# Three more x2 transposes in front of each group's logits, and VectorE's first weight splits held until two gathers are issued

## The chip, the cores and the metric

The kernel runs on one core of a Trainium2 chip. The metric is the device time in microseconds (us) of one execution, lower is better. The profiled execution is a single one of these, with every instruction recorded.

## What is computed

The reference chains three blocks. Their sizes set the work: 1536 tokens of width 512, 8 experts, hidden width 1024.

```python
attn = attention_with_hash_buckets(q, k, v, proj)          # (2, 8, 768, 64)
x    = attn.transpose(0, 2, 1, 3).reshape(1536, 512)
# layer 0: one expert per token, cosine router
logits = normalized(x) @ normalized(expert_emb).T / tau
x2[mask_e] = gate * (relu(x[mask_e] @ w1[e]) @ w2[e])
# layer 1: two experts per token, noisy router
logits = x2 @ w_gate
noisy  = logits + log1p(exp(x2 @ w_noise)) * noise
out[mask_e,k] += gate_k * (relu(x2[mask_e] @ w1[e]) @ w2[e])   # top 2
```

## The kernel before

The program has one instruction stream per engine, written out by hand, and the engines meet in semaphores. The order of work is the order of the code; no scheduler moves anything.

After attention, x lies in SBUF (`x_sb`) and is stored to DRAM as `x_tokens`. VectorE (DVE) then computes the routing of layer 0 in a row of small dependent operations. Their last result is `ids` (L886), the table that says which token rows each expert's tiles hold. It increments `routed`.

**Experts.** `experts(L)` exists once on each engine. For each expert e the tokens are handled as a macro tile of 2 tiles of 128 tokens in layer 0 and 3 in layer 1 (`MTS = (2, 3)`), with a loop over rest tiles where an expert has more tokens. GpSimd (POOL) gathers the rows of each tile from DRAM with one indirect DMA per tile (`gather`, L365, into `xm`). TensorE (PE) transposes a tile (4 matmuls against `ident`, L1203), ScalarE (ACT) copies the result as the high part `xTm_hi` (L569), DVE subtracts to get the low part `xTm_lo` (L897). PE then does the up product (L1249, 96 matmuls), ACT and DVE take the hidden values out as `hT_hi` (L592) and `hT_lo` (L928), and PE does the down product (L1231, 24 matmuls a tile).

**Weights.** Each expert's weights come in 8 chunks of 512 KB (`NCH = 8`): 0 to 3 are w1, 4 to 7 are w2. SP loads a chunk into a ring of 4 buffers `raw` (`RING = 4`, L295). ACT rounds it into `w_hi`, DVE subtracts the rest into `w_lo`, both 128x1024. SP may load chunk G only when both have finished chunk G - 4:

```python
if G >= RING:
    sp.wait_ge(split_hi, G - RING + 1)
    sp.wait_ge(split_lo, G - RING + 1)
sp.dma_start(raw_slot(c), chunk_src(w1, w2, e, c)).then_inc(raw_in[c % RING], 16)
```

Expert 0 of layer 0 is split on its own. ACT makes chunks 0 to 3 at L560, during the routing, and chunks 4 to 7 only behind its two `xTm_hi` copies (L581). DVE makes the low parts of chunks 0 to 3 by `first_low(range(NC1))` (L973) right after the gate table (L994), then the two `xTm_lo` parts, then `first_low` of chunks 4 to 7. From there on each `macro` splits the chunks of the next expert between its evacuations: two chunks, one `hT` part, four times (L581 and L592 on ACT, L918 and L928 on DVE).

**Routing of layer 1.** SP loads the 12 tiles of x2 (256 KB each, L308) into `x_sb`, on a semaphore of its own each (`x2_in[t]`). PE transposes tile t into bank t % 4 of PSUM (L1172, 4 matmuls); from tile 4 on it waits for DVE to be done with tile t - 4 (`rx_ev`). ACT copies it to `x2T_hi` (L631), DVE subtracts into `x2T_lo` (L827). When a group of 4 tiles is complete (`LG = 4`, so three groups), PE computes its logits (`logits`, L1149 x4 and L1152 x4) once `rx_ev` says that the group's last low part is there; ACT copies them out as `logT` (`logits_out`, L624), and PE transposes these back (`logits_back`, L1160 x4). DVE sums all of it at L822 (`r_sum`), the head of the second routing. The buffers `x2T_hi` and `x2T_lo` are double: tile 8 and later, which are group 2, must wait on ACT until the logits of group 0 are done (`lg_ps`).

`keep_clock(n)` (L1140) puts n dummy transposes of `ident` on PE.

Of the kernel before, what the change touches and what calls it, by code (L numbers as in the profile page):

```python
# [15 lines left out]
def attention_moe_kernel(nc, qT, kT, v, proj, expert_emb, tau, m1_w1, m1_w2,  # L16
# [8 lines left out]
    N, DM = noise.shape[0], H * D  # L25
    QC = S // P
    HALF = QC // 2
    NT = N // P
# [6 lines left out]
    MTS = (2, 3)  # L35
# [3 lines left out]
    LG = 4  # L39
# [11 lines left out]
    with ctx:  # L51
# [12 lines left out]
        def sb(name, shape, dt=f32):  # L64
            t = at(name, shape, dt, place[0])
            place[0] += nbytes(shape, dt)
            return t

        def sem(name):
            return ctx.enter_context(nc.semaphore(name))  # L70
# [74 lines left out]
        xm = [sb(f"xm{h}", [P, DM]) for h in range(2)]  # L145
# [51 lines left out]
        rt_act, rt_pe = sem("rt_act"), sem("rt_pe")  # L197
        shift_ready, onehot_ready, slots_ready = sem("shift_ready"), sem("onehot_ready"), sem("slots_ready")
        w_ready, d12_ready = sem("w_ready"), sem("d12_ready")
        routed = sem("routed")  # L200
        raw_in = [sem(f"raw_in{i}") for i in range(RING)]
        split_hi, split_lo = sem("split_hi"), sem("split_lo")
        x2_in = [sem(f"x2_in{i}") for i in range(NT)]
# [124 lines left out]
        def _(pool):  # L328
# [29 lines left out]
            def wait(s, value):  # L358

                pool.wait_ge(s, value)  # L360
                if not isinstance(value, int):
                    pool.sem_inc(pool_pass, 1)

            def gather(dst, idx, rows, s):
                return g.indirect_dma_start(out=dst, out_offset=None, in_=rows,  # L365
                                            in_offset=bass.IndirectOffsetOnAxis(ap=idx, axis=0),
                                            bounds_check=N - 1, oob_is_err=False).then_inc(s, 16)

            def scatter(rows, idx, src, s):
                return g.indirect_dma_start(out=rows, out_offset=bass.IndirectOffsetOnAxis(ap=idx, axis=0),  # L370
# [3 lines left out]
            def experts(L, x_rows, y_rows):  # L374
                s, MT = LS[L], MTS[L]

                def column(e, h):
                    return (idx_m[e % 4] if e else ids)[:, h:h + 1]

                def macro_x(e, r0):  # L380
                    if e:
                        wait(s["xm_ps"], MT * e)
                        for h in range(MT if e > 4 else 0):
                            wait(s[f"ym_out{h}"], 16 * (e - 3))
                        g.tensor_copy(idx_m[e % 4][:, 0:MT], ids[:, bass.ds(r0 + MT * e, MT)]).then_inc(s["idx_m"], 1)
                        wait(s["idx_m"], e)
                    for h in range(MT):
                        gather(xm[h][:], column(e, h), x_rows, s[f"xm_in{h}"])

                def rest_x(k, r, col):  # L390
                    wait(s["xr_ps"], r + 1)
# [58 lines left out]
        def _(act):  # L450
# [176 lines left out]
            for t in range(NT):  # L627
                act.wait_ge(rx_ps, t + 1)
                if t >= 2 * LG:
                    act.wait_ge(lg_ps, t // LG - 1)  # L630
                a.activation(x2T_hi[t // LG % 2][:, :, t % LG * P:(t % LG + 1) * P],  # L631
                             ps[:, t % X2_BANKS, :].rearrange("p (k n) -> p k n", n=P), ACT.Copy).then_inc(rx_hi, 1)
                if t > LG and t % LG == 1:
                    logits_out(t // LG - 1)
            logits_out(NT // LG - 1)
            act.wait_ge(act_table, 2)
# [10 lines left out]
        def _(dve):  # L647
# [322 lines left out]
            def first_low(chunks):  # L970
                for c in chunks:
                    dve.wait_ge(split_hi, c + 1)
                    v_.tensor_tensor(w_lo[0][:, c, :], raw[:, c % RING, :], w_hi[0][:, c, :].bitcast(f32),  # L973
                                     ALU.subtract).then_inc(split_lo, 1)
# [17 lines left out]
            link(v_.reciprocal(gates[:, 0, :], r_s[:]))  # L992
            wide = lambda gate: gate.unsqueeze(2).to_broadcast([P, NT, NX])
            v_.tensor_tensor(gate_tab[:], r_oh[0][:], wide(gates[:, 0, :]), ALU.mult).then_inc(g_ready, 1)  # L994
            first_low(range(NC1))

            experts(0)
# [31 lines left out]
        def _(pe):  # L1029
# [108 lines left out]
            def keep_clock(n):  # L1138
                for _ in range(n):
                    te.transpose(ps[:, 0, 0:P], ident[:], ident[:])  # L1140

            def routing(L):
# [13 lines left out]
                def logits_back(gr):  # L1156

                    pe.wait_ge(lg_ev, gr + 1)
                    for t in range(LG * gr, LG * (gr + 1)):
                        last = te.transpose(ps[:, LOGIT, t * 4 * NX:(t + 1) * 4 * NX], logT[:, t * P:(t + 1) * P],  # L1160
                                            ident[0:4 * NX, 0:4 * NX])
                    last.then_inc(logit_ps, 1)

                if L:
                    keep_clock(44)
                    pe.wait_ge(gate_split, 2)
                    for t in range(NT):
                        pe.wait_ge(x2_in[t], 16)
                        if t >= X2_BANKS:
                            pe.wait_ge(rx_ev, t - X2_BANKS + 1)  # L1170
                        for kk in range(KD):
                            last = te.transpose(ps[:, t % X2_BANKS, kk * P:(kk + 1) * P], x_sb[:, t, kk * P:(kk + 1) * P], ident[:])  # L1172
                        last.then_inc(rx_ps, 1)
                        if t and t % LG == 0:
                            logits(t // LG - 1)
                        if t > LG and t % LG == 2:
                            logits_back(t // LG - 1)
                    logits(NT // LG - 1)
                    logits_back(NT // LG - 1)

                pe.wait_ge(onehot_ready, L + 1)
# [155 lines left out]
```

## Time and profile before

| | us |
|---|---|
| median of 3 runs | 912.56 |
| lowest and highest | 909.87, 912.6 |
| profiled execution, its own time | 911.48 |
| span in its trace | 909.7 |

| engine | busy share of the span |
|---|---|
| TensorE | 90% |
| VectorE | 57% |
| ScalarE | 47% |
| GpSimd | 27% |

The mean granted clock of TensorE in the profiled execution was 0.956 of full speed. The profile names an instruction by its engine and its line in the kernel, the tile that it writes and the one that it reads. "Idle before, releaser" is the time in which the engine stood still ahead of the instruction and the instruction of another engine, or the transfer, that let it go on. The chain of waits is the path through the whole run that ended last. Places in the run are given in us from the span's start.

### The profile page before, as it was taken

To read this page: it belongs to the slowest core of one execution; us is meant where nothing else is said; L and a number is where in the kernel's file an instruction comes from. 1 tells how busy PE (TensorE), PEld (TensorE's weight loads), DVE (VectorE), ACT (ScalarE), POOL (GpSimd) and SP (SyncE) were. 2 spreads that over 40 slices of the span, in tenths; PEclk is the share of its full clock that TensorE was granted. 3 is DMA by queue.
4 is the path that set the end of the run, shared out by engine and by line. 5 is a ranking of instruction groups with operands and counts; after the bars stand their busy time and mean duration, and the time that the engine had idled before them with its cause. 6 is when DMAs were issued, how large, how long until landed. Compare 5 with 4: busy or idle time off the path is not lost.

```text
span 909.7 us, 12779 instructions
## 1 busy us (share of the span) xinstructions
PE 819.3 (90%) x4652; PEld 660.1 (73%) x4652; DVE 520.7 (57%) x884; ACT 423.4 (47%) x689; POOL 248.5 (27%) x247
## 2 busy tenths in 40 slices
PE   4899999999993589999999734999999999999996
PEld 2566566666661579999999623979798997889795
DVE  4788778877865666666666256626253653446221
ACT  5667677787775255555444131415152442425110
POOL 2000000000000313434433001645353664437231
PEclk9899999999997599999999985999999999999999
DMA  5414322130001476766665501725344754355110
GB/s 180 173 70 146 111 73 91 49 119 21 25 1 70 156 266 234 232 231 231 226 228 188 182 1 37 255 74 174 125 133 160 252 175 154 111 186 175 42 43 35
DMA packets 50041, 123.64 MB, mean 136 GB/s; under 512 B 10337, under 2 KB 12385, under 8 KB 49712
## 3 DMA queue, kind: packets, MB, share of 16 engines
q1 hardware_dynamic: 35488, 87.21, 29.0%
q0 software_dynamic: 12032, 29.02, 9.7%
q10 hardware_dynamic: 2448, 6.46, 1.9%
q8 instruction: 44, 0.72, 0.3%
q14 instruction: 29, 0.24, 0.1%
HBM read 109.34 MB, written 17.92 MB: 140 GB/s over the span
## 4 chain that ended last, share of the span: by engine, by line
PE 82%; DVE 8%; DMA 3%; ACT 3%; issue 2%; POOL 1%; ACTq 0%; POOLq 0%; SPq 0%; DVEq 0%
PE ps L1231 27%; PE ps L1249 24%; PE ps L1053 8%; PE ps L1076 7%; PE ps L1062 6%; PE ps L1275 3%; PE ps L1203 2%; PE ps L1043 2%; PE ps L1089 2%; DMA raw<-in_moe_w 1%; DVE row_low L721 1%; DMA xm<-x_tokens,ids 1%; DVE oh_lo L880 1%; ACT probs L473 1%; DVE w_lo L973 1%
## 5 line engine op out<-in xcount | busy, mean ns | idle before, releaser
L581 ACT ACTIVATE w_hi<-raw 128x1024 fp32r<-128x1024 f32 x124 | 129.1, 1055 | 94.4 <-PE ps L1231 75.5
L918 DVE TENSOR_TENSOR w_lo<-raw,w_hi 128x1024 fp32r<-128x1024 f32 x120 | 145.4, 1225 | 39.6 <-ACT w_hi L581 34.0
L1249 PE MATMUL ps<-xTm_hi,w_hi 128*128 128x256 f32 (+1 forms) x512 | 159.9, 312 | 2.9 <-ACT xTm_hi L569 2.9
L1249 PE MATMUL ps<-xTm_lo,w_hi 128*128 128x256 f32 (+1 forms) x512 | 159.6, 312 | 0.0
L1249 PE MATMUL ps<-xTm_hi,w_lo 128*128 128x256 f32 (+1 forms) x512 | 159.6, 312 | 0.0
L1231 PE MATMUL ps<-w_hi,hT_hi 128*128 128x512 f32 x320 | 128.9, 403 | 2.7 <-DVE hT_lo L928 2.7
L1231 PE MATMUL ps<-w_hi,hT_lo 128*128 128x512 f32 x320 | 125.7, 393 | 0.0
L1231 PE MATMUL ps<-w_lo,hT_hi 128*128 128x512 f32 x320 | 125.3, 392 | 0.0
L721 DVE TENSOR_REDUCE row_low<-ps 128x1 f32<-128x768 f32 x96 | 91.7, 956 | 46.6 <-PE ps L1053 45.8
L1053 PEld LDWEIGHTS ps<-K,Q 128*128 128x128 f32 (+1 forms) x384 | 68.2, 198 | 64.1 <-issue 35.9
L473 ACT ACTIVATE probs<-ps,exp_in 128x768 f32<-128x768 f32 x96 | 95.1, 991 | 22.0 <-DVE exp_in L725 22.0
L1053 PE MATMUL ps<-K,Q 128*128 128x512 f32 (+3 forms) x384 | 97.2, 377 | 8.4 <-DMA Q<-row_bits_Q 4.0
L1249 PEld LDWEIGHTS ps<-xTm_hi,w_hi 128*128 128x128 f32 x512 | 98.9, 193 | 4.1 <-ACT xTm_hi L569 3.5
L365 POOL DMA_INDIRECT xm<-x_tokens,ids x5 | 7.0, 1409 | 346.3 <-DVE ids L886 345.4
L1249 PEld LDWEIGHTS ps<-xTm_lo,w_hi 128*128 128x128 f32 x512 | 98.7, 193 | 0.5
L1249 PEld LDWEIGHTS ps<-xTm_hi,w_lo 128*128 128x128 f32 x512 | 98.7, 193 | 0.0
L480 ACT ACTIVATE probsT<-ps 128x512 f32<-128x512 f32 x96 | 57.0, 594 | 55.5 <-PE ps L1062 54.4
L1062 PE MATMUL ps<-ident,probs 128*128 128x128 f32 x576 | 81.9, 279 | 0.8 <-ACT probsT L480 0.6
L569 ACT ACTIVATE xTm_hi<-ps 128x512 fp32r<-128x512 f32 x40 | 23.9, 598 | 123.4 <-PE ps L1203 123.4
L592 ACT ACTIVATE hT_hi<-ps 128x384 fp32r<-128x384 f32 (+1 forms) x96 | 50.3, 524 | 65.4 <-PE ps L1249 58.7
L1076 PE MATMUL ps<-probsT,v 128*64 128x384 f32 x384 | 80.0, 514 | 0.0
L1062 PEld LDWEIGHTS ps<-ident,probs 128*128 128x128 f32 x576 | 65.8, 142 | 15.4 <-issue 14.3
(227 smaller groups left out, 1137.2 us busy)
## 6 DMA issues: line engine op xcount, KB each, us to landing
raw<-in_moe_w SPq DMA_DIRECT2D x128, 512.0 KB
rows_K<-in_k SPq DMA_DIRECT2D x8, 768.0 KB, 4.4
rows_Q<-in_q SPq DMA_DIRECT2D x8, 768.0 KB, 5.8
v<-in_v SPq DMA_DIRECT2D x8, 384.0 KB, 3.5
out<-xr ACTq DMA_DIRECT2D x1, 3072.0 KB, 14.6
x_tokens<-x_sb ACTq DMA_DIRECT2D x2, 1536.0 KB, 5.1
x_sb<-x_tokens SPq DMA_DIRECT2D x12, 256.0 KB, 5.1
K<-row_bits_K SPq DMA_DIRECT2D x24, 24.0 KB
```

What stands on the lines that cost most here:

```text
L473: a.activation(probs[s % 2][:], ps[:, sc:sc + 2, :].rearrange("p a n -> p (a n)")[:, 0:S], ACT.Exp, bias=exp_in[:, s % 2, 1:2], scale=exp_ ...
L480: a.activation(probsT[hf][:, 0:NA, head, cq * P:(cq + 1) * P], ps[:, PTA, 0:NA * P].rearrange("p (c n) -> p c n", n=P), ACT.Copy).then_inc ...
L581: a.activation(w_hi[E % 2][:, c, :], raw[:, c % RING, :], ACT.Copy).then_inc(split_hi, 1)
L592: a.activation(hT_hi[:, FC * i:FC * (i + 1), 0:TW], ps[:, n % UP_BANKS, 0:FC * TW].rearrange("p (k n) -> p k n", n=TW), ACT.Relu).then_inc ...
L721: v_.tensor_reduce(lows[:, 1:2], ps[:, sc:sc + 2, :].rearrange("p a n -> p (a n)")[:, 0:S], AX.X, ALU.min)\
L918: v_.tensor_tensor(w_lo[E % 2][:, c, :], raw[:, c % RING, :], w_hi[E % 2][:, c, :].bitcast(f32), ALU.subtract).then_inc(split_lo, 1)
L1053: last = te.matmul(ps[:, bank, 0:hi - lo], opd[a_][b][0:rows, head, cq * P:(cq + 1) * P], opd[b_][b][0:rows, head, lo:hi], start=(i == 0), ...
L1062: last = te.transpose(ps[:, bank, i * P:(i + 1) * P], probs[s % 2][:, kc * P:(kc + 1) * P], ident[:])
L1076: last = te.matmul(ps[head * D:(head + 1) * D, OB, 0:HALF * P], vv[b][:, head, kc, :], probsT[hf][:, kc, head, :], start=(kc == 0), stop=( ...
L1231: last = te.matmul(ps[:, bank, :], x_[:, fc, cols], w_[par][:, c, w], start=(fc == 0 and i == 0), stop=(fc == KF - 1 and i == 2))
L1249: last = te.matmul(ps[:, n % UP_BANKS, j * TW:(j + 1) * TW], w_[par][:, kk, f], x_[:, kk, 0:TW], start=(kk == 0 and m == 0), stop=(kk == K ...
L1275: last = te.matmul(ps[:, H0 + hf, :], x_[:, kk, :], w_[par][:, kk, w], start=(kk == 0 and i == 0), stop=(kk == KD - 1 and i == 2))
```

## The change

Two places are edited. First, in the routing of layer 1, `logits(0)` and `logits(1)` are issued behind the transposes of tiles 6 and 10 instead of 4 and 8, and the results of the first two groups are transposed back later; the last group's calls stay at the end, behind them. ACT's `logits_out` of group 0 comes behind its copy of tile 7 instead of 5, of group 1 behind 11 instead of 9. Second, in layer 0, the two indirect DMAs of expert 0 increment a new semaphore `x_issued` by one each through `engine_sem`, and DVE waits for 2 of them ahead of `first_low(range(NC1))`.

```diff
@@ semaphores @@
-        routed = sem("routed")
+        routed, x_issued = sem("routed"), sem("x_issued")
@@ GpSimd @@
-            def gather(dst, idx, rows, s):
+            def gather(dst, idx, rows, s, issued=None):
                 return g.indirect_dma_start(out=dst, out_offset=None, in_=rows,
                                             in_offset=bass.IndirectOffsetOnAxis(ap=idx, axis=0),
-                                            bounds_check=N - 1, oob_is_err=False).then_inc(s, 16)
+                                            bounds_check=N - 1, oob_is_err=False, engine_sem=issued).then_inc(s, 16)
...
-                        gather(xm[h][:], column(e, h), x_rows, s[f"xm_in{h}"])
+                        gather(xm[h][:], column(e, h), x_rows, s[f"xm_in{h}"], x_issued if e == L == 0 else None)
@@ ScalarE @@
-                if t > LG and t % LG == 1:
+                if t > LG and t % LG == LG - 1:
                     logits_out(t // LG - 1)
@@ VectorE @@
             v_.tensor_tensor(gate_tab[:], r_oh[0][:], wide(gates[:, 0, :]), ALU.mult).then_inc(g_ready, 1)
+            dve.wait_ge(x_issued, MTS[0])
             first_low(range(NC1))
@@ TensorE @@
                         last.then_inc(rx_ps, 1)
-                        if t and t % LG == 0:
+                        if t > LG and t % LG == 2:
                             logits(t // LG - 1)
-                        if t > LG and t % LG == 2:
-                            logits_back(t // LG - 1)
+                        if t > 2 * LG and t % LG == 1:
+                            logits_back(t // LG - 2)
                     logits(NT // LG - 1)
+                    logits_back(NT // LG - 2)
                     logits_back(NT // LG - 1)
```

The first order listing is TensorE's, in the routing of layer 1, from the transposes of x2 tile 4 (`x2_in4`) on. Before:

```order
L1172 MATMUL ps<-ident,x_sb 128x128 [waits rx_ev,x2_in4]
L1172 MATMUL ps<-ident,x_sb 128x128 x3
L1149 MATMUL ps<-x2T_hi_154,gate_hl 32x512 [waits rx_ev]
L1149 MATMUL ps<-x2T_hi_154,gate_hl 32x512 x3
L1152 MATMUL ps<-x2T_lo_156,gate_hl 16x512 x4
L1172 MATMUL ps<-ident,x_sb 128x128 [waits rx_ev,x2_in5]
L1172 MATMUL ps<-ident,x_sb 128x128 x3
L1172 MATMUL ps<-ident,x_sb 128x128 [waits rx_ev,x2_in6]
L1172 MATMUL ps<-ident,x_sb 128x128 x3
L1160 MATMUL ps<-ident,logT 128x32 [waits lg_ev]
L1160 MATMUL ps<-ident,logT 128x32 x3
```

The same stretch of TensorE in the changed kernel, whose lines are one higher there:

```order
L1173 MATMUL ps<-ident,x_sb 128x128 [waits rx_ev,x2_in4]
L1173 MATMUL ps<-ident,x_sb 128x128 x3
L1173 MATMUL ps<-ident,x_sb 128x128 [waits rx_ev,x2_in5]
L1173 MATMUL ps<-ident,x_sb 128x128 x3
L1173 MATMUL ps<-ident,x_sb 128x128 [waits rx_ev,x2_in6]
L1173 MATMUL ps<-ident,x_sb 128x128 x3
L1150 MATMUL ps<-x2T_hi_154,gate_hl 32x512 [waits rx_ev]
L1150 MATMUL ps<-x2T_hi_154,gate_hl 32x512 x3
L1153 MATMUL ps<-x2T_lo_156,gate_hl 16x512 x4
L1173 MATMUL ps<-ident,x_sb 128x128 [waits rx_ev,x2_in7]
L1173 MATMUL ps<-ident,x_sb 128x128 x3
```

Tiles 5 and 6 now stand ahead of the first group's logits, and the first `logits_back` has moved out of this stretch, behind the transposes of tile 9.

On VectorE, behind the gate table of layer 0, the order before was:

```order
L994 TENSOR_TENSOR gate_tab<-r_oh_171,gates 128x96 [waits dve_step]
L973 TENSOR_TENSOR w_lo_112<-raw,w_hi_110 128x1024 [waits split_hi] x4
L897 TENSOR_TENSOR xTm_lo<-ps,xTm_hi 128x4x128 [waits xm_hi_l0] x2
L973 TENSOR_TENSOR w_lo_112<-raw,w_hi_110 128x1024 [waits split_hi] x4
L918 TENSOR_TENSOR w_lo_113<-raw,w_hi_111 128x1024 [waits split_hi] x2
```

It is now:

```order
L994 TENSOR_TENSOR gate_tab<-r_oh_171,gates 128x96 [waits dve_step]
L973 TENSOR_TENSOR w_lo_112<-raw,w_hi_110 128x1024 [waits split_hi,x_issued]
L973 TENSOR_TENSOR w_lo_112<-raw,w_hi_110 128x1024 [waits split_hi] x3
L897 TENSOR_TENSOR xTm_lo<-ps,xTm_hi 128x4x128 [waits xm_hi_l0] x2
L973 TENSOR_TENSOR w_lo_112<-raw,w_hi_110 128x1024 [waits split_hi] x4
```

Nothing is reordered on VectorE; the first of the eight splits has one wait more.

## Rows read from the trace of the kernel before

**Rows 1.** The chain that ended last, shares of the span by engine.

```profile
PE 82%; DVE 8%; DMA 3%; ACT 3%; issue 2%; POOL 1%; ACTq 0%; POOLq 0%; SPq 0%; DVEq 0%
```

**Rows 2.** Stretches: us, PE, PEld, DVE, ACT, POOL busy, granted clock, DMA share, GB/s.

```profile
340.00:506.00 166.00, 166.00 (x1073) 151.15 (x1072) 101.42 (x110) 78.67 (x96) 65.02 (x61) 1.00 0.66 220
306.00:311.00 5.00, 1.05 (x6) 0.81 (x7) 0.69 (x1) 0.60 (x1) 0.00 (x0) 0.72 0.96 348
516.00:520.00 4.00, 3.12 (x14) 2.59 (x15) 2.06 (x4) 1.79 (x3) 0.00 (x0) 0.57 1.01 361
```

**Rows 3.** Timeline of GpSimd, gathers of both layers: start, us, instruction, idle before.

```profile
301.16 2.22 POOL L365 DMA_INDIRECT xm<-x_tokens,ids  x1 [295.11 <-DVE ids L886]
303.69 1.77 POOL L365 DMA_INDIRECT xm<-x_tokens,ids  x1 [0.31 <-issue]
...
315.74 1.96 POOL L365 DMA_INDIRECT gate_r<-gates,ids  x1 [0.30 <-issue]
...
562.15 1.00 POOL L365 DMA_INDIRECT xm<-x_tokens,ids  x1 [0.30 <-issue]
```

**Rows 4.** Timeline of VectorE, the eight splits of expert 0.

```profile
301.10 4.62 DVE L973 TENSOR_TENSOR w_lo<-raw,w_hi 128x1024 fp32r<-128x1024 f32 x4
...
313.33 4.63 DVE L973 TENSOR_TENSOR w_lo<-raw,w_hi 128x1024 fp32r<-128x1024 f32 x4 [0.25 <-ACT w_hi L581]
```

**Rows 5.** Timeline of TensorE, the head of expert 0 and of layer 1's first.

```profile
310.61 1.11 PE L1203 MATMUL ps<-ident,xm 128*128 128x128 f32 x4 [3.20 <-DMA xm<-x_tokens,ids]
313.18 0.55 PE L1249 MATMUL ps<-xTm_hi,w_hi 128*128 128x256 f32 x1 [1.46 <-ACT xTm_hi L569]
...
565.88 0.66 PE L1203 MATMUL ps<-ident,xm 128*128 128x128 f32 x4 [0.59 <-DMA xm<-x_tokens,ids]
```

**Rows 6.** Timeline of the SP queue: chunk 4 of expert 0, chunk 0 of expert 1.

```profile
302.40 0.37 SPq L295 DMA_DIRECT2D raw<-in_moe_w  x1
...
314.63 0.34 SPq L295 DMA_DIRECT2D raw<-in_moe_w  x1
```

**Rows 7.** Timeline of ScalarE: the first splits behind the gathers and behind new chunks.

```profile
312.25 3.88 ACT L581 ACTIVATE w_hi<-raw 128x1024 fp32r<-128x1024 f32 x4
319.47 1.06 ACT L581 ACTIVATE w_hi<-raw 128x1024 fp32r<-128x1024 f32 x1 [3.33 <-DMA raw<-in_moe_w]
```

**Rows 8.** The chain in order of time, 303 to 344: start, us, what.

```profile
303.69 6.88 DMA xm<-x_tokens,ids
...
318.04 6.11 DMA raw<-in_moe_w
...
334.16 0.61 DVE hT_lo L928
```

**Rows 9.** Timeline of TensorE in the routing of layer 1.

```profile
516.32 2.78 PE L1172 MATMUL ps<-ident,x_sb 128*128 128x128 f32 x12 [1.23 <-DMA x_sb<-x_tokens]
519.66 1.16 PE L1149 MATMUL ps<-x2T_hi,gate_hl 128*32 128x512 f32 x4 [0.56 <-DVE x2T_lo L827]
...
521.59 1.03 PE L1172 MATMUL ps<-ident,x_sb 128*128 128x128 f32 x8
...
525.77 1.11 PE L1149 MATMUL ps<-x2T_hi,gate_hl 128*32 128x512 f32 x4 [0.97 <-DVE x2T_lo L827]
...
531.82 1.11 PE L1149 MATMUL ps<-x2T_hi,gate_hl 128*32 128x512 f32 x4 [1.41 <-DVE x2T_lo L827]
```

**Rows 10.** Timelines there of ScalarE (first row) and VectorE (second).

```profile
522.22 0.60 ACT L631 ACTIVATE x2T_hi<-ps 128x512 fp32r<-128x512 f32 x1 [2.48 <-PE ps L1172]
...
535.00 0.56 DVE L822 TENSOR_REDUCE r_sum<-ps 128x192 f32<-128x384 f32 x1 [3.24 <-PE ps L1160]
```

**Rows 11.** The loads of x2: the SP queue's issues, and issue to landing.

```profile
511.00 5.85 SPq L308 DMA_DIRECT2D x_sb<-x_tokens  x12
...
DMA to landing us min/median/max: 2.7/5.1/5.8
```

**Rows 12.** The low parts of x2 on VectorE, all 12.

```profile
L827 DVE TENSOR_TENSOR x2T_lo<-ps,x2T_hi x12: 680/692/692, 515.1 to 531.1; 128x512 fp32r<-128x512 f32 x12
```

## The prediction

> **What bounds the kernel now.** I read the chain of waits first: TensorE carries 82% of it [rows 1], so time is to be had only where TensorE stands still. A stretch table shows that it does not from 340 to 506, where it is busy for 166.00 of 166.00 us [rows 2]. What starts earlier by some us at 340 therefore ends earlier by as much at 506, and the reverse. The two edits lie in the two gaps around this stretch, and each can be worked out alone.
>
> *Gap A, 300 to 344, head of expert 0.* GpSimd issues the two gathers at 301.16 and 303.69 and takes 2.22 and 1.77 us for them; the same instruction takes 1.00 at the head of layer 1 [rows 3]. What differs is VectorE, which runs four splits of 1.16 us each beside them from 301.10 to 305.72 [rows 4]; in layer 1 it has no split to do there. The first split also frees a ring slot, so SP issues chunk 4 at 302.40 [rows 6], ahead of the second gather. From 306 to 311 the DMA engines are 96% busy at 348 GB/s [rows 2], and the second gather, issued at 303.69, lands 6.88 us later [rows 8]. TensorE waits 3.20 us for it and starts the up product only at 313.18 [rows 5].
> That start isn't what ends the gap. ScalarE makes chunks 4 to 7 behind its `xTm_hi` copies, from 312.25 [rows 7]; VectorE follows at 313.33 [rows 4]; only then may SP load expert 1 (314.63, [rows 6]). The chain goes through these loads, one of them 6.11 us long, to the `hT_lo` part at 334.16 that the down product needs [rows 8]. So the gap's length is set by when chunks 4 to 7 are split.
>
> *Gap B, 511 to 535, routing of layer 1.* Three times TensorE stands before a group's logits waiting for the low part of the group's last tile: 0.56, 0.97 and 1.41 us [rows 9]. Only then does it do the logits and the next transposes, so ScalarE and VectorE stand still meanwhile: ScalarE 2.48 us ahead of tile 5 [rows 10]. Each engine waits in turn. The end is `r_sum` at 535.00 [rows 10].
>
> **The change, part A.** No instruction is added but one wait. The gathers now run beside small operations only, so I take the layer 1 price, 1.00 each with 0.31 between [rows 3]: they end at 302.2 and 303.5 instead of 303.4 and 305.5. The splits start at about 303.6 instead of 301.1: **2.5 us later**, the price. Queued behind them are the two `xTm_lo` parts and chunks 4 to 7 on VectorE, and SP, which waits for the first split with chunk 4 (now about 304.9).
> Landing: the last gather of layer 1's head ended its issue at 563.15 [rows 3] and its tile was transposed from 565.88 on [rows 5], 2.7 us later. That puts the second gather at 306.2 instead of 310.56. Its transposes take up to 1.11 [rows 5], its copy 0.60, so ScalarE is free for chunk 4 at about 307.9 instead of 312.25. VectorE ends the first splits at 308.2 and the `xTm_lo` parts at 309.6, where TensorE starts the up product: 3.6 us earlier.
> But chunk 4 is late next. The nearest load, chunk 0 of expert 1, took 4.84 us from issue (314.63) to ScalarE's start (319.47) [rows 6, 7]. By that chunk 4 lands at 309.7 and shifts by -2.55, not -4.4. Chunk 7, issued about 3.4 us behind chunk 4, lands at 313.1, or some 0.6 later because expert 1's gathers (two of 256 KB at 348 GB/s are 1.5 us of transfer) now fall among these loads. ScalarE and VectorE need 1.06 and 1.16 us on it: 316.0 instead of 317.96, so -2. The chain runs through the load that this frees (318.04), and with fewer gathers beside it that load should take less than 6.11. Taking -2 for the chunk and 0.4 for the lighter queue, **A = -2.4 us**. Bounds: -4 if chunk 4 lands as soon as ScalarE is free, -0.5 if the gathers stay slow (below).
> The earlier start of the up product is worth nothing by itself: TensorE then waits longer for `hT_lo`.
>
> **Part B.** The same 96 matmuls, in another order; 12 tiles stay 12 tiles. Worked out from tile 4 on, whose transposes end at 519.1 as before [rows 9]:
> - Tiles 5 and 6 need low parts 1 and 2, long done, and their loads. Their issues are 0.49 us apart from 511.00 and land 5.1 us later in the median, 5.8 at most [rows 11]; tile 6 lands at about 519. TensorE runs at half clock here (0.57 from 516 to 520, [rows 2]), and a tile costs 0.9, at full clock 0.52 (8 matmuls in 1.03, [rows 9]). Both end at 520.3.
> - Logits 0 need low part 3 (519.6): no wait. They take 2.0 (519.66 to the next transposes at 521.59), to 522.3. Meanwhile ScalarE and VectorE do tiles 5 and 6; that is the gain.
> - Tiles 7, 8, 9 follow to 523.6; ScalarE copies tile 7 at 522.9, `logT` at 523.4, then 8 and 9. TensorE waits 0.4 for `logT`, transposes back (0.43), does tile 10 and reaches logits 1 at 524.9; low part 7 was done at 524.2. They end at 526.9, tile 11 at 527.3.
> - ScalarE and VectorE add 0.60 and 0.69 [rows 10, 12] with the small gaps before: low part 11 at 528.7. TensorE waits 1.4 for it. This last wait stays, since nothing is left to put in front.
> - Logits 2 end at 530.8, `logT` at 531.4, and the transposes back at 531.9; those of group 1 hide under that copy. `r_sum` starts at 531.9 instead of 535.00: **B = -3.1 us**.
> Bounds: -3.8 if tiles 5 and 6 go at full clock, -1.3 if logits 0 stay at half clock, where 4 matmuls of 512 columns take twice the 1.1 us (+1.8).
>
> **A rule that speaks against the change.** The slow gathers stand beside VectorE's two-input subtractions [rows 3, 4]. The Trainium skill (SBUF — State Buffer, Who interferes with whom) says that `tensor_tensor` takes only the shared pair's read interface and infers that it doesn't stall descriptor generation, which needs the write interface. By it the gathers would be slow for a reason of their own, and the sum would be that of the first rival.
>
> **Sum.** A -2.4, B -3.1: -5.5 us. From the profiled execution's own time, 911.48, that is 906.0. The median of the runs shown is 1.1 us above that execution and the lowest 1.6 below; I keep the sum.
>
> **The rivals.**
> 1. *The gathers are slow by themselves*, for instance since they are the first of the program. For it: those of layer 1 come when the code has long been run. Against it: the indirect DMA of `gate_r` at 315.74, no longer the first, takes 1.96 beside the splits of [rows 4], on a table of 8 values a row [rows 3]. They would end at 305.46 as now, the splits would start there, 4.4 later, chunk 4 would land at 306.75 + 4.84 = 311.6 against 312.25, and A would be -0.6: 907.8.
> 2. *The clock takes part of B.* The half-clock stretch around 516 to 520 [rows 2] ends later, or a new one comes in gap A's longer wait for `hT_lo`. One group of logits at half clock costs 1.8, two such stretches 3.6: 908 to 909.6.
> 3. *Slower: the wait lasts until the gathers have landed*, and they land no sooner than now. VectorE starts at 310.6, chunk 4 is issued at 311.8 and lands at 316.7, or 317.9 with 6.11; against 312.25 A is +4.4 to +5.7, with B +1.3 to +2.6: 912.8 to 914.1. It decides from the point where the splits start behind 309.2 (A above +3.1). Against it: the semaphore is attached to the issuing engine, and without the ring's loads in front nothing holds the gathers up.
> 4. *The reordering does nothing*, since the loads of x2 are the limit. Against it: the last is issued at 516.4 and landed by 522.2 [rows 11], 5 us ahead of its new use at 526.9. B = 0 would give 909.1.
>
> **How the numbers follow.** The forecast gets 0.72 (its own range 903.8 to 908.0), rival 1 0.10, rival 2 0.10, rival 3 0.03, rival 4 0.05. About 0.3% (2.7 us) is what a measurement of this kernel tells from no change. Faster by more than that: the forecast, rival 1 and half of rivals 2 and 4, 0.89; within it their other halves and a part of rival 3, 0.09; slower, rival 3 with a stretch at half clock on top, 0.02. Range 903.3 to 909.3: A and B at their favourable bounds less a little for the spread of the runs, up to rival 4.
>
> **What would show it.** Right: two gathers of about 1.0 us, the first split at 303.6, the up product at about 309.6, chunks 4 to 7 now waiting on ScalarE for their loads, `hT_lo` at about 331.8; in the second gap one wait of some 1.4 us left before logits, and `ids` to `r_sum` shorter by 3. Wrong: gathers still of 2 us, a first split behind 305, TensorE waiting for `x_sb` loads behind tile 4, or a granted clock of 0.5 at the first logits.

## The result and the profile after

| us | before | change |
|---|---|---|
| first comparison, median (lowest to highest) | 911.21 (909.35 to 912.6) | 901.68 (901.49 to 903.07) |
| median of all runs of the study (84 and 21) | 910.4 | 902.4 |
| profiled execution, its own time | 911.48 | 901.77 |
| span in its trace | 909.7 | 899.9 |
| mean granted clock of TensorE | 0.956 | 0.964 |

The first comparison gave a ratio of 0.990 with an interval of 0.9875 to 0.9925; two later ones of the unchanged files gave 0.9921 (0.9897 to 0.9945) and 0.9917 (0.9885 to 0.9949). The change is worth about -8 us. Both 902.4 and the 901.68 of the first comparison lie below the forecast range of 903.3 to 909.3.

The chain that ended last, shares of the span by engine, of the change:

```profile
PE 82%; DVE 8%; DMA 3%; issue 2%; ACT 2%; POOL 1%; ACTq 0%; SPq 0%; POOLq 0%; DVEq 0%
```

The shares are those of before [rows 1] but for ScalarE's, 2% for 3%; they don't show where the gain lies. That is read from the two gaps. The head of expert 0, GpSimd's timeline:

```profile
299.77 1.19 POOL L365 DMA_INDIRECT xm<-x_tokens,ids  x1 [293.72 <-DVE ids L886]
301.27 1.00 POOL L365 DMA_INDIRECT xm<-x_tokens,ids  x1 [0.31 <-issue]
...
309.44 1.13 POOL L365 DMA_INDIRECT gate_r<-gates,ids  x1 [0.30 <-issue]
```

VectorE's, from the same point (first split, fourth `hT_lo` part), and behind it `r_sum` of the second gap:

```profile
302.31 4.63 DVE L973 TENSOR_TENSOR w_lo<-raw,w_hi 128x1024 fp32r<-128x1024 f32 x4 [2.52 <-DMA xm<-x_tokens,ids]
...
328.98 0.68 DVE L928 SCALAR_TENSOR_TENSOR hT_lo<-ps,hT_hi 128x512 fp32r<-128x512 f32 x1
...
525.50 0.56 DVE L822 TENSOR_REDUCE r_sum<-ps 128x192 f32<-128x384 f32 x1 [3.23 <-PE ps L1161]
```

The SP queue's issue of chunk 4:

```profile
303.62 0.37 SPq L295 DMA_DIRECT2D raw<-in_moe_w  x1
```

ScalarE, which now waits for the chunks themselves:

```profile
307.40 1.06 ACT L581 ACTIVATE w_hi<-raw 128x1024 fp32r<-128x1024 f32 x1 [1.48 <-DMA raw<-in_moe_w]
...
311.78 1.06 ACT L581 ACTIVATE w_hi<-raw 128x1024 fp32r<-128x1024 f32 x1 [0.29 <-DMA raw<-in_moe_w]
```

TensorE, the transposes of the second gathered tile and the first up matmul:

```profile
304.62 0.66 PE L1205 MATMUL ps<-ident,xm 128*128 128x128 f32 x4 [0.62 <-DMA xm<-x_tokens,ids]
...
308.24 0.36 PE L1251 MATMUL ps<-xTm_hi,w_hi 128*128 128x256 f32 x1 [2.96 <-DVE xTm_lo L897]
```

The gathers cost 1.19 and 1.00 us instead of 2.22 and 1.77 [rows 3], and TensorE waits 0.62 instead of 3.20 for the second tile [rows 5]. The indirect DMA of `gate_r` cost 1.13 instead of 1.96, although VectorE has splits beside it here too (from 308.49 to 311.04).

Times from the span's start can't be compared between traces as they stand: `ids` falls at 300.07 in the trace of before and at 298.68 here, and over all traces at 297.0 to 300.1 where nothing ahead of it is edited. So from here on places in the first gap are counted from `ids`, and those in the second from "the last y", the `ym` (L912) by which VectorE takes out the last down product of layer 0 (499.98 in the trace of the change). Between the two, from expert 1's up product to the last y, every trace of either kernel has 162.85 to 162.94 us.

TensorE in the second gap, of the change:

```profile
509.59 4.53 PE L1173 MATMUL ps<-ident,x_sb 128*128 128x128 f32 x20 [0.51 <-DMA x_sb<-x_tokens]
513.77 1.34 PE L1150 MATMUL ps<-x2T_hi,gate_hl 128*32 128x512 f32 x4
...
515.87 1.47 PE L1173 MATMUL ps<-ident,x_sb 128*128 128x128 f32 x12
517.62 0.43 PE L1161 MATMUL ps<-ident,logT 32*128 32x32 f32 x4 [0.28 <-ACT logT L624]
517.98 0.66 PE L1173 MATMUL ps<-ident,x_sb 128*128 128x128 f32 x4
518.39 1.16 PE L1150 MATMUL ps<-x2T_hi,gate_hl 128*32 128x512 f32 x4
...
522.33 1.11 PE L1150 MATMUL ps<-x2T_hi,gate_hl 128*32 128x512 f32 x4 [1.41 <-DVE x2T_lo L827]
```

Of the three waits for low parts, 0.56, 0.97 and 1.41 us [rows 9], the last is left, as forecast.

### The profile page after: what moved, and what is told of

Its sections match the earlier page's. It is cut to its first block, busy times and chain, and to the rows that moved or that the text cites. A ratio compares the mean times of both kernels' runs of the same rounds, so it can differ in the third digit from the quotient of the medians.

```text
span 899.9 us, 12780 instructions
## 1 busy us (share of the span) xinstructions
PE 814.1 (90%) x4652; PEld 655.8 (73%) x4652; DVE 521.1 (58%) x884; ACT 424.2 (47%) x689; POOL 243.9 (27%) x247
## 4 chain that ended last, share of the span: by engine, by line
PE 82%; DVE 8%; DMA 3%; issue 2%; ACT 2%; POOL 1%; ACTq 0%; SPq 0%; POOLq 0%; DVEq 0%
PE ps L1233 27%; PE ps L1251 24%; PE ps L1054 8%; PE ps L1077 7%; PE ps L1063 6%; PE ps L1277 3%; PE ps L1044 2%; PE ps L1205 2%; DMA raw<-in_moe_w 2%; PE ps L1090 2%; DVE row_low L721 1%; PE ps L1173 1%; DVE oh_lo L880 1%; DVE w_lo L973 1%; DMA xm<-x_tokens,ids 1%
## 5 line engine op out<-in xcount | busy, mean ns | idle before, releaser
L365 POOL DMA_INDIRECT xm<-x_tokens,ids x5 | 5.2, 1049 | 341.7 <-DVE ids L886 340.8
```

## The experiments

Each was built on one of the two kernels and profiled once. Logits 0 are the first four matmuls of L1149 (L1150 in the change). The times by part, in us:

| kernel | `ids` to 4th `hT_lo` | `hT_lo` to expert 1's up | last y to logits 0 | logits 0 to `r_sum` | `r_sum` to `ids` of layer 1 |
|---|---|---|---|---|---|
| before | 34.00 | 9.74 | 13.00 | 15.34 | 23.49 |
| e3, before again | 34.35 | 8.14 | 12.76 | 15.72 | 23.49 |
| e8, dummies | 34.33 | 8.13 | 12.36 | 16.73 | 23.48 |
| e10, idle wait | 34.35 | 8.15 | 12.53 | 15.50 | 23.10 |
| e2, order only | 34.58 | 8.14 | 12.53 | 11.59 | 23.48 |
| e1, wait only | 32.22 | 9.73 | 12.29 | 16.57 | 23.09 |
| e5, load held | 32.69 | 9.72 | 12.56 | 16.60 | 23.50 |
| e6, wait for one | 31.02 | 8.14 | 12.90 | 15.33 | 23.09 |
| e7, wait for landing | 33.87 | 9.68 | 12.80 | 18.22 | 23.10 |
| after | 30.30 | 8.13 | 13.79 | 11.73 | 23.09 |
| e4, change again | 30.26 | 9.67 | 13.15 | 11.59 | 23.09 |
| e9, change again | 31.17 | 8.15 | 13.51 | 11.60 | 23.10 |
| e16, change again | 29.93 | 8.14 | 13.77 | 11.58 | 23.11 |
| e12, splits on GpSimd | 30.03 | 9.67 | 12.89 | 11.60 | 23.09 |
| e11, 66 dummies | 32.70 | 9.77 | 12.51 | 11.59 | 23.10 |
| e15, 66 dummies | 30.51 | 8.34 | 13.05 | 11.57 | 23.12 |
| e13, four in front | 31.18 | 8.16 | 14.04 | 8.98 | 23.12 |
| e14, four and 66 | 30.76 | 8.13 | 13.67 | 8.97 | 23.10 |

### The two halves and the repeats: e1 to e4, e9, e16

e1 has the second edit alone: `x_issued`, its two increments and VectorE's wait. e2 has the first alone: the order of `logits`, `logits_back` and `logits_out`. e3 is the kernel before, and e4, e9 and e16 the change, unedited.

> VectorE's wait for the two gathers alone, TensorE's order as before. Counted from ids (L886), so that drift ahead of it doesn't enter. Theory 1 (the two edits are independent and the first is worth more than I gave it): hT_lo's last part of expert 0 comes 30.4 us behind ids instead of 34.1, the routing of layer 1 keeps its 28.3 us, and the time falls by 4 to 6 us. Theory 2 (the first edit is worth the 2.4 us of the prediction and the rest is drift of the run): hT_lo at 31.7 behind ids or the time falls by 2 to 3 us only.

> TensorE's and ScalarE's new order in the routing of layer 1 alone. Theory 1 (as predicted): from the last ym (L912) of layer 0 to r_sum 25.5 us instead of 28.3, the stretch from ids to expert 1's up product unchanged at 43.9, the time falls by 2.5 to 3.5 us. Theory 2 (the order gives only what the clock allows): 26.5 us or more where TensorE is at half clock in front of the first logits, a fall of under 2 us.

> The kernel before, profiled once more, as a measure of what one trace differs from the next. If the 1.39 us by which ids came earlier in the changed kernel's trace is drift of TensorE's clock in the attention part, ids lands anywhere between 298.5 and 300.5 here; if it belongs to the change, it lands at 300.1 again. The gathers take 2.2 and 1.8 us again, and the half-clock stretch at expert 0's down product shows whether it is there every time.

> The changed kernel, profiled once more. Theory 1 (the 1.6 us between hT_lo and expert 1's up product belong to the change, since TensorE's wait falls otherwise): TensorE at full clock from 329 to 337 again, expert 1's up product 8.2 us behind hT_lo. Theory 2 (chance of the clock): a stretch at half clock there, 9.8 us. ids to expert 1's up product 38.6 by the first, up to 40.2 by the second.

> The changed kernel in many runs, since four runs stand against twelve of each half. The halves alone gave -3.9 and -4.3 us. Theory 1 (they add up): -8.2, a median of 902.3 where the kernel before has 910.5. Theory 2 (together they give more, for instance since the clock falls less): under 901.5.

> The changed kernel again. By the sum of the parts seen in the traces (hT_lo 3.0 earlier behind ids, the routing of layer 1 4.1 shorter, the pause at r_w 0.4) it is 7.5 us below the kernel before, a ratio of 0.992; if the first comparison (0.990) was right, 9 us. hT_lo 30.3 to 32.7 behind ids, first logits to r_sum 11.6.

Measured, medians: e1 906.65 against 910.52, ratio 0.996 (0.9941 to 0.9979), so -3.9. e2 906.26, 0.9958 (0.9938 to 0.9978), -4.3. Together -8.2, the change's -8: the two halves add up. Each median is beyond the forecast of its half (-2.4 and -3.1), but the intervals, -5.4 to -1.9 and -5.7 to -2.0, take in both forecasts. Of e1's two theories neither fits whole: the time fell by nearly the 4 us of the first, while `hT_lo` came 32.22 behind `ids`, later than either had it. e2 beat its first theory: from the last y to `r_sum` 24.12 instead of 25.5. e3 took 908.93 and e4 900.55, once each; single runs say little, since those of before in the same comparison go from 907.0 to 914.04. e9 had a median of 902.84 against 909.92, e16 903.16 against 909.43, as the sum of the halves had it.

The repeats show what one trace can't. Before's own logits 0 to `r_sum` varies from 15.33 to 16.73, once 18.22, in traces with nothing changed there. The clock makes most of it. In the four long traces (e1, e5, e7, e8: 16.57 to 18.22) the last four matmuls of L1149 take 1.91 or 1.92 us, in the four short ones (15.33 to 15.72) 1.11 or 1.12. This is e1's trace. First its timeline, then its stretch around that point (PE, PEld, DVE, ACT, POOL busy, granted clock, DMA share, GB/s):

```profile
526.23 1.91 PE L1150 MATMUL ps<-x2T_hi,gate_hl 128*32 128x512 f32 x4 [1.41 <-DVE x2T_lo L827]
```

```profile
526.00:528.00 2.00, 1.77 (x5) 0.72 (x6) 0.18 (x1) 0.00 (x0) 0.00 (x0) 0.50 0.00 0
```

The same four matmuls took 1.11 in [rows 9]. In the new order this part is 11.6 to 11.7 in every trace that has it.

### Why the gathers were slow: e5 and e6

Two things leave the gathers' neighbourhood when VectorE waits: its splits, and SP's load of chunk 4, which the first split frees. e5 keeps the splits where they were in before and holds the load instead; e6 waits for one gather only. Both, and e7 below, keep the old order in the second gap.

```diff
# e5: the kernel before, with x_issued, and in SP's loads
+                if G == RING:
+                    sp.wait_ge(x_issued, MTS[0])
# e6: against the change
-            dve.wait_ge(x_issued, MTS[0])
+            dve.wait_ge(x_issued, 1)
```

> VectorE's splits start at once as before, but SP issues chunk 4 only when both gathers are issued. Computation unchanged. Theory 1 (most of the gain of the first edit is that the gathers stand ahead of the ring's loads): the gathers still take 2.2 and 1.8 us to issue beside the splits, the second tile is transposed at about 8.2 us behind ids (10.5 before, 6.0 changed), chunk 4 is issued at 5.5 behind ids against 4.9, hT_lo comes at 30.8 to 31.3, and the time falls by nearly as much as with VectorE's wait alone. Theory 2 (it is the gathers' faster issue that counts): the second tile stays later than 9.5 behind ids, hT_lo at 33 or later, a fall of 1 us or none.

> VectorE waits for the first gather's issue only. Theory 1 (splits slow whatever gather they run beside): the first gather takes 1.2 us, the second 1.8 again; the splits start 2.3 behind ids instead of 3.6, chunk 4 is issued 1.3 us earlier; the second tile is transposed at about 7.5 to 9 behind ids. hT_lo at 29.5 to 31, since chunk 4's landing sets it. Theory 2 (a gather behind ring loads is what hurts): second tile at 10 behind ids again, and hT_lo at 33 or more.

GpSimd's timeline of e6:

```profile
299.72 1.19 POOL L365 DMA_INDIRECT xm<-x_tokens,ids  x1 [293.67 <-DVE ids L886]
301.22 1.83 POOL L365 DMA_INDIRECT xm<-x_tokens,ids  x1 [0.31 <-issue]
```

The first gather, without splits beside it, is the fast one; the second, beside them, is slow, in one and the same run. In e5 the loads are held and the splits run as before:

```profile
299.76 2.21 POOL L367 DMA_INDIRECT xm<-x_tokens,ids  x1 [293.71 <-DVE ids L888]
302.28 1.78 POOL L367 DMA_INDIRECT xm<-x_tokens,ids  x1 [0.31 <-issue]
```

So the issue of the two gathers is slowed by the splits, not by the loads, and not by their being the first. The inference weighed in the prediction (the Trainium skill, SBUF — State Buffer, Who interferes with whom: `tensor_tensor` leaves the write interface free, hence descriptor generation) doesn't hold for this pair: the indirect DMAs pay 1.03 and 0.77 us beside the splits. The price isn't the same for every one. This gather of before stands wholly beside the splits of 313.33 to 317.96 [rows 4], and it paid 0.24:

```profile
314.20 1.24 POOL L365 DMA_INDIRECT xm<-x_tokens,idx_m  x1 [0.30 <-issue]
```

What sets the price, no run here tells.

The landing is another matter. TensorE's transposes of the second tile, in e5:

```profile
306.38 1.11 PE L1205 MATMUL ps<-ident,xm 128*128 128x128 f32 x4 [1.43 <-DMA xm<-x_tokens,ids]
```

They start 7.71 behind `ids` instead of 10.54 in before and 5.94 in the change. The issues of e5 are as slow as before's, so 2.8 of the 4.6 us by which the second tile comes earlier are had by keeping the ring's loads from going out ahead of it, and 1.8 by the faster issues.

For the time, e6 had a median of 906.48, ratio 0.997 (0.9948 to 0.9992), the same as e1: one waited-for gather is enough, with `hT_lo` at 31.02. e5 had 908.74 against 909.92, 0.9984 (0.9962 to 1.0007), which can't be told from no change, although its `hT_lo` comes at 32.69, 1.6 earlier than before. So its first theory was right on the gathers and the second tile, its second on the time.

### What the delay of the splits costs: e7

Here, on the kernel before, VectorE waits until both gathers have landed:

```diff
+            for h in range(MTS[0]):
+                dve.wait_ge(LS[0][f"xm_in{h}"], 16)
```

> VectorE waits until both gathers have landed, not only until they are issued (the third rival's mechanism, by itself). Theory 1 (hT_lo follows chunk 4's issue one for one): the splits start at about 5.9 behind ids instead of 3.6, chunk 4 goes out 2.3 us later, hT_lo at 32.6 and a gain of 1.5 to 2 us over the kernel before. Theory 2 (as the third rival had it, later than before): hT_lo above 34.3 and a time above the kernel before's.

The first split starts 6.01 behind `ids` instead of 3.63, `hT_lo` comes at 33.87, and the median is 913.26, ratio 1.002 (0.9992 to 1.0047). The 2.4 us took back the whole gain; that they cost more than that isn't clear of the noise. Neither theory fits whole: `hT_lo` is later than the first had it (32.6) and earlier than the second (34.3), and the gain of 1.5 to 2 us isn't there. ScalarE's timeline shows the price, a wait for chunk 4:

```profile
310.51 1.06 ACT L581 ACTIVATE w_hi<-raw 128x1024 fp32r<-128x1024 f32 x1 [3.81 <-DMA raw<-in_moe_w]
```

Its trace also has the longest second gap, 18.22, where no edit was made. By its parts up to `hT_lo` e7 should be near the kernel before; why the median of ten runs lies 3.3 above it is open.

### The clock ahead of expert 1: e8

From `hT_lo` to expert 1's up product the traces show 8.1 or 9.7 us, but for e15's 8.34. Stretches in the down product, of before, of the change and of e4:

```profile
336.00:338.00 2.00, 2.00 (x8) 1.71 (x7) 0.56 (x1) 0.60 (x1) 0.00 (x0) 0.50 0.80 264
```

```profile
330.00:332.00 2.00, 2.00 (x12) 1.64 (x12) 0.47 (x2) 0.60 (x1) 0.00 (x0) 1.00 0.93 313
```

```profile
330.00:332.00 2.00, 2.00 (x8) 1.61 (x8) 0.20 (x1) 0.00 (x0) 0.00 (x0) 0.50 0.95 338
```

The change and e4 are the same file: after the wait for `hT_lo` the granted clock is at its full 2.4 GHz in one and at 1.2 GHz in the other. e8 puts dummies into before's waits there:

```diff
+                            if E == 0 and h == 0 and fc in (4, 6):
+                                for _ in range(4 if fc == 4 else 20):
+                                    te.transpose(ps[:, YR, 0:P], ident[:], ident[:])
```

> The kernel before with 4 and 20 dummy transposes of ident into an idle bank, where TensorE waits for the third and fourth hT_lo of expert 0 (some 0.5 and 2.2 us). From hT_lo to expert 1's up product the traces so far show either 8.14 or 9.7 us, in kernels with and without the change. Theory 1 (it is the clock, which falls in that wait in some executions): the granted clock stays at 1.00 through the down product and the stretch is 8.1. Theory 2 (something else): 9.7 at full clock. No theory gives more than 1.6 us of the whole.

The part took 8.13, at clock 1.00, and e8 took 909.99 in its one run against a median of 912.13. But e3 and e10 reach 8.14 and 8.15 without dummies. So the run agrees with the dummies keeping the clock and doesn't show it. The 1.6 us difference that the first pair of traces has here goes with the clock, which either kernel has at either level, and is no part of the change's worth.

### A pause that moved: e10

In the change, `r_sum` to `ids` of layer 1 is 23.09 instead of 23.49, with no edit there. VectorE, before and then after:

```profile
536.37 0.21 DVE L1002 TENSOR_SCALAR r_w<-r_u 128x96 f32<-128x96 f32 x1 [0.81 <-ACT r_u L639]
```

```profile
526.48 0.21 DVE L1003 TENSOR_SCALAR r_w<-r_u 128x96 f32<-128x96 f32 x1 [0.42 <-ACT r_u L639]
```

e10 adds to before one wait that is met already, ahead of `first_low(range(NC1))`:

```diff
+            dve.wait_ge(routed, 1)
```

> The kernel before, with a wait on VectorE at the place of the new one, on a semaphore that is long there (routed, 1). From r_sum to ids of layer 1 the kernels with a wait at that place took 23.09 us and those without 23.49. Theory 1 (one more instruction moves VectorE's later code, and a pause in front of r_w goes with it): 23.09 here too, the gathers slow as before (2.2 and 1.8 us), hT_lo at 34. Theory 2 (the 0.4 comes from the earlier state of the engines): 23.49.

23.10, with everything else as before; its one run took 908.0. In before, e2, e3, e5 and e8, where VectorE's instructions are as they were, it is 23.48 to 23.50; wherever one wait or two were added, 23.09 to 23.12. e12, below, adds none and has four splits fewer on VectorE, and there it is 23.09 too. So it isn't the waiting: one instruction more or four fewer far ahead takes 0.4 off a pause some 225 us later. That those behind it then lie at other addresses would fit; no run here settles it.

### Moving splits to GpSimd: e12

On the change, GpSimd makes the four low parts ahead of its wait for the stores of `x_tokens`, during the routing, and VectorE's wait and its first four splits go:

```diff
+            for c in range(NC1):
+                wait(split_hi, c + 1)
+                g.tensor_tensor(w_lo[0][:, c, :], raw[:, c % RING, :], w_hi[0][:, c, :].bitcast(f32),
+                                ALU.subtract).then_inc(split_lo, 1)
...
-            dve.wait_ge(x_issued, MTS[0])
-            first_low(range(NC1))
```

ScalarE's splits of chunks 4 to 7 stand ahead of its wait for the gate table.

> The changed kernel, but GpSimd makes the low parts of chunks 0 to 3 during the routing of layer 0, when it has nothing to do, and ScalarE makes chunks 4 to 7 ahead of the gate table. VectorE's first four splits and its wait go. Theory 1 (gap A is the ring of four buffers turning): chunks 4 to 7 are loaded 10 us or more before ids, expert 1's loads start at about 10 behind ids instead of 10.7 to 12, and hT_lo at 26 to 29, until TensorE's own work (13.9 for the up product behind 8.2) becomes the bound; a gain of 2 to 5 us over the changed kernel. Theory 2 (GpSimd's subtractions hold VectorE's routing up, or are so slow that they hold the gathers up): ids later by more than 2 us counted from the last row maximum, or the first gather later than 1.1 behind ids, and no gain.

909.54 against 912.13 is 0.9975 (0.9949 to 1.0001), so most of the gain of the change is gone, as its second theory had it. `hT_lo` came 30.03 behind `ids`, no earlier than in the change, where the first theory had 26 to 29. First GpSimd, then VectorE beside it:

```profile
285.62 9.24 POOL L446 TENSOR_TENSOR w_lo<-raw,w_hi 128x1024 fp32r<-128x1024 f32 x4 [279.56 <-ACT w_hi L564]
```

```profile
285.95 2.05 DVE L668 TENSOR_SCALAR r_s<-r_nrm 128x12 f32<-128x12 f32 x1
288.03 0.23 DVE L669 RECIPROCAL r_s<-r_s 128x12 f32<-128x12 f32 x1
...
290.33 2.26 DVE L671 TENSOR_TENSOR r_s<-r_s,r_nrm 128x12 f32<-128x12 f32 x1
...
294.92 0.17 DVE L985 TENSOR_SCALAR r_nrm<-r_nrm 128x12 f32<-128x12 f32 x1
```

Four operations on 12 elements a partition take 2.00 to 2.26 us beside GpSimd's, 0.17 once it is done, and `ids` comes 7.9 us later (23.51 behind the row of sums `r_ssq`, against 15.62). So it goes both ways: VectorE's splits slow GpSimd's gathers, and GpSimd's splits hold up VectorE. That VectorE shares a pair of ports with GpSimd is what the same section of the Trainium skill describes, and this trace agrees.

### The clock at the second gap: e11 and e15

The new order starts logits 0 later, behind two more tiles. `keep_clock(44)` became `keep_clock(66)`; e11 and e15 are the same file.

> The changed kernel with 66 dummy transposes instead of 44 ahead of the routing of layer 1, which fills 2.3 us more of TensorE's wait for the first tile of x2. Theory 1 (the half-clock stretch that sets in while TensorE waits for x2 is what B varies by): TensorE is at full clock through the first logits, from the last ym to r_sum 24.1 us (the best seen) instead of 24.7 to 25.5, and 0.5 to 1.4 us off the median. Theory 2 (the later wait, for tile 2, drops the clock anyway, or the dummies hold the first transposes up): 24.7 or more, no gain.

> The changed kernel with 66 dummy transposes once more, in more runs. Theory 1: the first logits start 12.5 us behind the last ym instead of 13.2 to 13.8, so 0.5 to 1.3 us below e16, the changed kernel on the same chip. Theory 2 (the one trace at 12.5 was chance, as the kernels before had it too): no difference from e16.

901.54 and 901.33, ratios 0.9877 (0.9822 to 0.9932) and 0.99 (0.9872 to 0.9928); beside e15 on the same chip the change had 903.16. Last y to logits 0 was 12.51 and 13.05 against 13.15 to 13.79 in four traces of the change. By the stretch from 508 to 510 of the change's trace, the clock is down while it waits for x2:

```profile
508.00:510.00 2.00, 1.49 (x7) 1.09 (x7) 0.95 (x2) 1.19 (x2) 0.00 (x0) 0.50 0.98 345
```

The direction fits, but the intervals overlap, and e2 (12.53) and e12 (12.89), with the new order and 44 dummies, start logits 0 as early: a gain of up to 1 or 2 us, not settled.

### Taking the last wait away too: e13 and e14

The change has three tiles in front of the logits of groups 0 and 1, where before had one (so two more, not three as the title has it), and none in front of group 2's. It leaves 1.41 us ahead of the last logits. e13 puts one more tile in front of the logits of groups 0 and 1, and all three `logits_back` behind the last logits; e14 has 66 dummies as well.

```diff
-                        if t > LG and t % LG == 2:
+                        if t > LG and t % LG == LG - 1:
                             logits(t // LG - 1)
-                        if t > 2 * LG and t % LG == 1:
-                            logits_back(t // LG - 2)
                     logits(NT // LG - 1)
+                    logits_back(NT // LG - 3)
```

> The changed kernel with one more tile in front: logits of group 0 behind tile 7, of group 1 behind tile 11, and the results transposed back only behind the last logits. Theory 1 (it is the order): tile 11's low part is made while TensorE does the logits of group 1, so the last wait of 1.41 us ahead of the logits of group 2 goes, and the first transposes back are off the path as well. First logits start 0.5 us later, first logits to r_sum 9.3 us instead of 11.6: 1.5 to 2 us off the changed kernel. Theory 2 (ScalarE, which may copy tiles 8 and later only behind the first logits, becomes the bound): tile 11's low part is still late, and the sum changes by less than 0.5.

> The same with 66 dummy transposes ahead of the tiles of x2 instead of 44. Theory 1 (the clock): from the last ym to the first logits 13.0 us instead of up to 14.3, at full clock, and 0.5 to 1 us less than e13 in the median. Theory 2: no difference.

TensorE in e13:

```profile
515.69 1.18 PE L1150 MATMUL ps<-x2T_hi,gate_hl 128*32 128x512 f32 x4
...
517.65 1.91 PE L1173 MATMUL ps<-ident,x_sb 128*128 128x128 f32 x16
519.32 1.18 PE L1150 MATMUL ps<-x2T_hi,gate_hl 128*32 128x512 f32 x4
...
521.49 1.11 PE L1150 MATMUL ps<-x2T_hi,gate_hl 128*32 128x512 f32 x4
...
523.46 1.18 PE L1161 MATMUL ps<-ident,logT 32*128 32x32 f32 x12
```

No row waits: the logits of group 1 now fill the 1.41 us in which VectorE makes the last low part. Logits 0 to `r_sum` is 8.98 instead of 11.6, while logits 0 starts about 0.5 later than in the change (14.04 against a mean of 13.56 in its four traces). The median is 900.34, 0.9883 (0.9854 to 0.9912), against the change's 903.16 on the same chip. e14 had 898.58, 0.9878 (0.9843 to 0.9913), the lowest median of the study, 4.6 below the change's on the same chip and 3.8 below that of all the change's runs. Its interval and e13's overlap almost wholly, and e13's overlaps a little with the change's own of 0.9885 to 0.9949; what carries the verdict on the fourth tile is the part from logits 0 to `r_sum`, 8.98 and 8.97. Whether the 66 dummies add to it isn't shown.

## Why the prediction was wrong, by its steps

The direction was right, and so was each of the two mechanisms in the main. Two terms of the sum were too small, the loads behind chunk 4 in gap A and the time that gap B had before. Means over traces, against the forecast, in us:

| term | forecast | measured | from |
|---|---|---|---|
| A, gap of expert 0 | -2.4 | -3.3 | 34.3 (5 traces without a wait or held load) to 31.0 (9 with the full wait) |
| B, second gap | -3.1 | -4.0 | 28.9 (8 with the old order) to 24.9 (6 with the new, 44 dummies) |
| `r_w`'s pause | none | -0.4 | 23.5 to 23.1 |
| sum | -5.5 | -7.7 | the medians say -8.0 |

B leans on e7's 18.22: without that trace the old order has 28.6, and B is -3.7.

The rest of the distance from 906.0 to 902.4 is the base: the profiled execution, at 911.48, lay 1.1 above the median of 84 runs. The first comparison's own difference, 9.5, is in turn 1.5 more than all runs together show, and part of that is luck. Between the spans of its two traces, 9.8 apart, A is -3.7, the clock ahead of expert 1 -1.6, B -2.8, `r_w`'s pause -0.4, and `ids` falls 1.4 earlier with no edit ahead of it. So in that pair B came out a little under the forecast, and 3.0 of the 9.8 us are no work of the change.

**Gap A, the front.** Counted from `ids`, the forecast had the first split at 3.5, chunk 4's issue at 4.8 and the up product at 9.5; they came at 3.63, 4.94 and 9.56. The gathers cost 1.19 and 1.00 against 1.00 each. Rival 1 (slow by themselves) is refuted by e6. Rival 3 (the wait lasts until landing) didn't happen, and e7 shows what it would have cost: the gain, with no clear loss.

**Gap A, the loads: the first step that failed.** "By that chunk 4 lands at 309.7." I took its landing from chunk 0 of expert 1, 4.84 us [rows 6, 7]; it took 3.78, from the issue at 303.62 to ScalarE's start at 307.40. That is 8.7 behind `ids` instead of 9.6, and it is 8.6 to 8.7 in all nine traces with the full wait: half the way to the favourable bound, where ScalarE is free (7.8). The load that chunk 7 frees, at 318.04 in before and 17.97 behind `ids`, went out 15.49 behind it, 2.5 earlier instead of 2. And the term of 0.4 for "the lighter queue" was too small. The chain of the change has these loads:

```profile
307.01 4.75 DMA raw<-in_moe_w
...
314.17 5.28 DMA raw<-in_moe_w
...
321.87 4.85 DMA raw<-in_moe_w
```

The last two, 5.28 and 4.85, stand where before had 6.11 [rows 8] and 5.25: 1.2 us where the forecast had 0.4. The two terms, 2.5 and 1.2, are the -3.7 of this pair. The loads vary: e5's chain has one of 6.97, and `hT_lo` with the full wait comes anywhere from 29.9 to 32.7. So how the 0.9 by which the mean -3.3 exceeds the forecast is shared between the two isn't known. The mean lies inside the bounds -4 to -0.5; I took too little of it.

**Gap B: the new order's time was right, the old one's was not.** Logits 0 were to start 0.6 later and did (12.65 to 13.27 in the means of traces that go from 12.29 to 13.79, so the agreement is in part luck). From there to `r_sum` I had 531.9 - 520.3 = 11.6, and six traces have 11.58 to 11.73. Three waits less one, the free start of logits 0 and 1, and the last 1.41 us all came as worked out. (Tiles 7 to 9 at 0.52 each end at 523.9, not 523.6; the wait for `logT` takes that up, and it was 0.28 instead of 0.4.) What failed is the value it was set against: 15.34 of the one trace is with e6's 15.33 the lowest of eight, whose mean is 16.25 (15.97 without e7), since in four of them the clock is down behind the old order's last wait (e1's last logits at 0.50). Rival 2 had the sign of this wrong: from logits 0 to `r_sum` the traces of the old order spread by 1.4 us (2.9 with e7's), those of the new by 0.16. The table's -4.0 is 4.65 less 0.62. Rival 4 is refuted by e2.

**The pause** was at nothing in the sum, and no row of before could tell of it; e10 shows that it goes with a wait that is met already. **The range** had 903.3 as its lower end, from A and B at their bounds. Nothing in it stood for the spread of before itself, neither that of its parts nor that of the base, and that is how -8 fell outside.

## What to carry to other kernels

Bulk work that is ready can cost more than it saves when it starts beside another engine's indirect DMAs: by slowing their issue, and by the loads that it lets go out ahead of them. Here a delay of 2.6 us at the start of the splits brought the step that depends on them forward by 3.3. Before a group's matmuls that need a neighbour's last result, put as many independent ones as the buffers allow, until no wait is left in front of them: three tiles in front instead of one gave 4 us, a fourth 2 to 3 more. And take the old value of a stretch with waits in it from several traces: one trace's clock can be 1 to 2 us off in each gap, as much as the edit is worth.

## What the hardware showed unexpectedly

- VectorE's fp32 `tensor_tensor` of 128x1024 slows GpSimd's issue of an indirect DMA: 1.19 against 2.21 us for the first gather, 1.00 against 1.77 to 1.83 for the second, but 1.24 for a later one beside such splits. VectorE's own four take 4.62 us beside the gathers and 4.63 without them in [rows 4] and the change's trace. GpSimd's own `tensor_tensor` holds VectorE's operations on 12 elements for 2.0 to 2.3 us, though not its reciprocal (0.23).
- TensorE's granted clock after a wait of 1 to 2 us differs from trace to trace: 8.1 or 9.7 us for the same down product in two traces of one file, and 15.3 to 18.2 for one routing stretch. `ids` of layer 0 falls anywhere within 3 us; what moves it wasn't traced.
- One wait instruction more on VectorE, or four splits fewer, shortened a pause of the same engine by 0.4 us, some 225 us later.
